# Half 0's strided scores in other banks, constants turned on TensorE, ScalarE's mix ahead of the exponentials, half 7's strided values in two parts

## The chip, the cores and the metric

The kernel runs on one core of a Trainium2 chip. The metric is the device time of one execution in microseconds (us); lower is better. Before and after are each given as the median of three runs on one chip. The engines are named as in the profile: PE is TensorE's matmul, PEld its weight load, DVE is VectorE, ACT is ScalarE, POOL is GpSimd, SP is SyncE, which here only issues transfers. All run their own instruction streams and meet at semaphores.

## What is computed

Sparse attention, then a channel mix, then a gated convolution, all in float32, over 4 batches of 576 tokens, 8 heads of 64:

```python
rel = pos[:, None] - pos[None, :]
mask_local = (rel >= 0) & (rel < 32)                                # heads 0-3
mask_strided = (rel >= 0) & (pos[None, :] % 32 == pos[:, None] % 32)  # heads 4-7
attn = softmax(where(mask, q @ k.T / 8, -1e9)); x = attn @ v        # (4, 576, 512)

x_prev = x shifted by one token
xk = mu_k * x + (1 - mu_k) * x_prev
xr = mu_r * x + (1 - mu_r) * x_prev
k = relu(xk @ w_k); r = sigmoid(xr @ w_r)
x = r * (k * k @ w_v)

h = relu(x @ w_in)                                                  # (4, 576, 1024)
out = (h * sigmoid(conv3(h, conv_w))) @ w_out
```

## The kernel before

A batch is worked in two halves of 288 tokens, so there are eight halves, h = 0 to 7 (NH = 8). Attention and mix of the halves are interleaved by a plan written out by hand: while PE does the mix of half h, it does the attention of half h + 1 in between. The mix of a half has 20 slots. Slots 0 to 7 are the tiles of x_k w_k, slots 8 to 11 those of x_r w_r, slots 12 to 19 the product with w_v, two slots for each of its four tiles. Half 0 multiplies plain float32; the later ones split each operand in a high and a low part and use three products for each (L663 to L665, and L714 to L716), so a tile is 12 matmuls of 288 columns. PLAN and SECOND (L67, L68) say in which slot of the mix PE does scores, ACT exponentials, DVE the normalization and PE the values: for the local block of the next half slots 1, 2, 4, 8, for the strided block 4, 5, 9, 12 (half 1: 2, 3, 5, 7 and 5, 6, 9, 11).

Each engine's program is one loop over halves and slots. In a slot PE first does the attention steps that stand there and then the mix (L746 to L751). Values and scores are very small matmuls: a strided block of an odd half is 88 matmuls in program order, each of which the chip runs as two, with a weight load each. The banks of tiles are a ring of four: tile t waits until ACT has done the ReLU of tile t - 4, that is `relu_done` at FT * h + t - 3 (L675). ACT does for each of the first eight tiles a ReLU, a square and the cast to the high part (L828, L832, L836), for the next four the sigmoid (L842). It also casts the mixed inputs (high_xk L848, high_xr L854) and does the exponentials (L817), one for each score tile, 9 in a local block, 11 in a strided one. ACT's functions lie in tables; where exponentials follow the sigmoids of the half before, a table is loaded (ACT_TABLE_LOAD). In ACT's loop (L897 to L916) the order in slot s is: exponentials, high_xr in slots 1 and 3, then the mix of tile s - 1.

The start stands outside the loops. PE warms up with matmuls of zeros (keep_warm, L720), turns q and k of half 0 (turn_rows), does the three score blocks (L730, L731, L734), the values (L736, L737, L741), and between the last of them the first products of the mix (plain_w_k, L649). DVE masks the scores and takes their maxima (mask_and_max, L1004), lays k out (lay_k, L1150), and turns the constants mu_k, mu_r and conv_w (rows_c to cols_c, L1163). ACT lays q out, and copies the strided values of half 0 (L894). The strided scores of half 0 are in banks 4 and 5 as the local ones are, so PE waits for the maxima of these (L533).

Transfers: SP issues, in this order, rows of q for half 0, V for the local heads, four loads of w_k of 512 KB each, rows of half 1, w_v and w_r, then the V rows of half 1 (L365 to L379). POOL issues the constants and 18 of the 24 loads of the strided V rows of half 0 (L461), ACT the other six (L884). At the end of the attention of half 7 POOL loads the next weights (L503) and SP x2 (L397); the gated convolution follows as a loop.

Of the kernel before, what the change touches and what calls it, by code (L numbers as in the profile page):

```python
# [10 lines left out]
P = 128  # L11
# [5 lines left out]
def attention_channel_mix_gated_conv(  # L17
# [17 lines left out]
    HG = H // 2  # L35
# [41 lines left out]
    WARM_START, WARM_COLS, WARM_SLOT = 23, 224, 4  # L77
# [14 lines left out]
    with ExitStack() as ctx:  # L92
# [32 lines left out]
        BW = 3  # L125
# [58 lines left out]
        const_loaded, const_turned = sem("const_loaded"), sem("const_turned")  # L184
# [16 lines left out]
        o_done, o_copied, first_copied = sem("o_done"), sem("o_copied"), sem("first_copied")  # L201

# [157 lines left out]
        def _(sp):  # L360
# [67 lines left out]
        def _(pool):  # L428
# [32 lines left out]
            load_v_strided(pool, 0, 0, range(1, HG))  # L461
# [60 lines left out]
        def _(pe):  # L522
            def scores(h, i):
# [9 lines left out]
                wait(pe, maxed, tiles_at(h, i) if h or kind == STR else 0)  # L533
# [20 lines left out]
            def values(h, i):  # L554
# [8 lines left out]
                if kind == STR and first == 0:  # L563
                    if h > 1:
                        wait(pe, vs_loaded[c], 16 * VS_DMAS * (h // 2))
                    else:
                        wait(pe, vs_first[c], 16 * (VS_DMAS if c else VS_DMAS - VS_DMAS // HG))
                        if not c:
                            wait(pe, vs_head, 16 * VS_DMAS // HG)
# [25 lines left out]
                else:  # L595
                    order = side_by_side(kind, first, tiles)
                    for two in (order[n:n + 2] for n in range(0, tiles, 2)):
# [13 lines left out]
                mm.then_inc(o_done, 1)  # L611

            def attention(h, slot):
                for i in of_slot(h, 3, slot):
                    values(h, i)
# [118 lines left out]
            scores(0, 2)  # L734
            keep_warm(2 * WARM_SLOT)
# [74 lines left out]
        def _(act):  # L810
# [76 lines left out]
            exps(0, 1)  # L887
            exps(0, 2)

            act.wait_ge(o_done, block_at(1))  # L890
            for pair in range(PAIRS):
                for which in range(2):
                    src, dst = strided_out(0, (pair,), which)
                    copied = nc.scalar.copy(dst, src)  # L894
                copied.then_inc(first_copied, 1)

            for h in range(NH):  # L897
                for slot in range(SLOTS):
# [7 lines left out]
                    if slot >= 1:  # L906
                        mlp(h, slot - 1)
# [65 lines left out]
        def _(dve):  # L973
# [74 lines left out]
            def attention(h, slot):  # L1048
                for i in of_slot(h, 3, slot):
                    copy_out(h, i)  # L1050
# [251 lines left out]
```

## Time and profile before

| | us |
|---|---|
| median of three runs | 531.36 |
| lowest, highest | 530.97, 531.49 |
| the profiled execution | 531.16 |
| its span, first to last instruction | 529.3 |
| PE busy | 517.5 |
| mean granted TensorE clock | 0.997 of full speed |

A profiled execution gives, for each instruction, when it started and how long it took, and what ended the idle time of its engine before it ("issue" where the engine waited for nothing that the profile shows). Lines L... are lines of the kernel before. Matmul durations overlap, since matmuls are pipelined.

### The profile page before, as it was taken

What the parts mean: (1) busy time and instruction counts of PE and PEld (TensorE: products, weight loads), DVE (VectorE), ACT (ScalarE), POOL (GpSimd) and SP (SyncE); (2) the same over time, 40 slices, a digit from 0 to 9 for tenths busy, and PEclk for the clock granted to TensorE, in tenths of its full rate; (3) what the DMA queues carried; (4) which work ended last, traced back from release to release, by engine and by line L of the source; (5) the groups of instructions that cost most, each with busy time, mean ns of one, the idle gap of its engine ahead of it and who ended that gap; (6) DMA issues with size and microseconds to landing.
All of it is one profiled execution on the core that took longest, in us unless ns stands there. A gap on an engine that the chain in (4) does not pass through costs nothing.

```text
span 529.3 us, 15349 instructions
## 1 busy us (share of the span) xinstructions
PE 517.5 (98%) x6200; PEld 480.2 (91%) x6203; DVE 325.3 (61%) x815; ACT 287.8 (54%) x783; POOL 119.3 (23%) x145
## 2 busy tenths in 40 slices
PE   7799999999999999999989999999999999999997
PEld 6477999999999999999989999988998899889985
DVE  5769985658658566657644745883397039807910
ACT  4389288296394592690970724761474048416720
POOL 9229972022031040140221682000000000000000
PEclk9999999999999999999998999999999999999999
DMA  9983423343243341332106126001300130010011
GB/s 203 191 276 56 72 76 63 65 94 65 62 90 65 94 70 41 82 63 45 48 2 249 46 80 213 4 0 61 109 1 12 68 109 0 19 61 0 0 40 59
DMA packets 98622, 39.07 MB, mean 74 GB/s; under 512 B 90952, under 2 KB 91134, under 8 KB 98558
## 3 DMA queue, kind: packets, MB, share of 16 engines
q1 hardware_dynamic: 93992, 33.09, 25.3%
q0 software_dynamic: 1824, 4.44, 2.6%
q10 hardware_dynamic: 2742, 0.66, 0.8%
q8 instruction: 44, 0.72, 0.6%
q14 instruction: 20, 0.16, 0.1%
HBM read 28.72 MB, written 9.44 MB: 72 GB/s over the span
## 4 chain that ended last, share of the span: by engine, by line
PE 85%; DVE 5%; ACT 3%; POOL 3%; issue 2%; DMA 1%; POOLq 0%; DVEq 0%; ACTq 0%
PE ps L769 19%; PE ps L779 19%; PE ps L663 8%; PE ps L664 8%; PE ps L665 8%; PE ps L714 6%; PE ps L715 6%; PE ps L716 6%; PE ps L608 2%; PE ps L550 2%; POOL vs L356 2%; ACT sm L817 2%; DMA vs<-in_v_dram 1%; PE ps L592 1%; DVE diff L1065 1%
## 5 line engine op out<-in xcount | busy, mean ns | idle before, releaser
L486 POOL TENSOR_TENSOR k_lo<-k,k_hi 128x288 fp32r<-128x288 f32 x64 | 60.9, 956 | 192.2 <-ACT k_hi L836 192.2
L1243 DVE SCALAR_TENSOR_TENSOR cbuf<-hbuf,cols_c,cbuf 128x576 f32<-128x576 f32 x64 | 52.4, 819 | 63.5 <-ACT cbuf L939 62.4
L714 PE MATMUL ps<-k_hi,wb_hi 128*128 128x288 f32 x256 | 76.8, 300 | 0.0
L715 PE MATMUL ps<-k_lo,wb_hi 128*128 128x288 f32 x256 | 76.2, 298 | 0.0
L716 PE MATMUL ps<-k_hi,wb_lo 128*128 128x288 f32 x256 | 76.1, 297 | 0.0
L663 PE MATMUL ps<-xk_hi,wa_hi 128*128 128x288 f32 x224 | 67.0, 299 | 0.0
L664 PE MATMUL ps<-xk_lo,wa_hi 128*128 128x288 f32 x224 | 66.1, 295 | 0.0
L665 PE MATMUL ps<-xk_hi,wa_lo 128*128 128x288 f32 x224 | 66.1, 295 | 0.0
L779 PE MATMUL ps<-wb_hi,g_hi 128*128 128x512 f32 x144 | 57.5, 399 | 0.0
L779 PE MATMUL ps<-wb_hi,g_lo 128*128 128x512 f32 x144 | 56.8, 394 | 0.0
L779 PE MATMUL ps<-wb_lo,g_hi 128*128 128x512 f32 x144 | 56.5, 392 | 0.0
L769 PE MATMUL ps<-x_hi,wa_lo 128*128 128x288 f32 x256 | 55.0, 296 | 0.0
L769 PE MATMUL ps<-x_hi,wa_hi 128*128 128x288 f32 x256 | 54.9, 296 | 0.0
L769 PE MATMUL ps<-x_lo,wa_hi 128*128 128x288 f32 x256 | 54.3, 293 | 0.0
L817 ACT ACTIVATE sm<-sm,nb 128x64 f32<-128x64 f32 (+1 forms) x160 | 52.1, 327 | 1.0 <-DVE nb L1009 0.9
L714 PEld LDWEIGHTS ps<-k_hi,wb_hi 128*128 128x128 f32 x256 | 48.9, 191 | 0.3
L715 PEld LDWEIGHTS ps<-k_lo,wb_hi 128*128 128x128 f32 x256 | 48.9, 191 | 0.1
L716 PEld LDWEIGHTS ps<-k_hi,wb_lo 128*128 128x128 f32 x256 | 48.7, 190 | 0.0
L854 ACT CAST xr_hi<-mixed 128x288 fp32r<-128x288 f32 x28 | 11.4, 431 | 62.9 <-DVE mixed L1086 62.9
L966 ACT COPY ob<-ps 128x512 f32<-128x512 f32 x18 | 10.6, 587 | 63.0 <-PE ps L779 62.9
L663 PEld LDWEIGHTS ps<-xk_hi,wa_hi 128*128 128x128 f32 x224 | 42.2, 188 | 0.9
L664 PEld LDWEIGHTS ps<-xk_lo,wa_hi 128*128 128x128 f32 x224 | 42.2, 188 | 0.0
(107 smaller groups left out, 1166.5 us busy)
## 6 DMA issues: line engine op xcount, KB each, us to landing
x2d<-x2s SPq DMA_DIRECT2D x8, 576.0 KB, 3.1
x2raw<-x2d SPq DMA_DIRECT2D x4, 1152.0 KB, 5.5
out_dram<-ob SPq DMA_DIRECT2D x16, 256.0 KB, 2.0
raw<-in_q_dram SPq DMA_DIRECT2D x96, 36.0 KB, 2.0
raw<-in_k_dram SPq DMA_DIRECT2D x96, 36.0 KB, 1.9
wk_raw<-in_moe_w_k_dram SPq DMA_DIRECT2D x4, 512.0 KB, 9.2
wv_raw<-in_moe_w_v_dram SPq DMA_DIRECT2D x4, 512.0 KB, 5.1
ws<-in_moe_w_in_dram POOLq DMA_DIRECT2D x4, 512.0 KB, 7.3
```

The lines of the kernel that those rows point to most:

```text
L486: nc.gpsimd.tensor_tensor(k2_lo[:, m], k2[:, m % K2RING], k2_hi[:, m].bitcast(F32), ALU.subtract).then_inc(k2_done, 1)
L663: nc.tensor.matmul(dst, w_hi(t), x_hi(t), start=(t == 0), stop=False)
L664: nc.tensor.matmul(dst, w_hi(t), x_lo(t), start=False, stop=False)
L665: mm = nc.tensor.matmul(dst, w_lo(t), x_hi(t), start=False, stop=(t == KT - 1))
L714: nc.tensor.matmul(dst, wb_hi[:, f, cols], k2_hi[:, f, :], start=(f == 0), stop=False)
L715: nc.tensor.matmul(dst, wb_hi[:, f, cols], k2_lo[:, f, :], start=False, stop=False)
L716: mm = nc.tensor.matmul(dst, wb_lo[:, f, cols], k2_hi[:, f, :], start=False, stop=(f == FT - 1))
L769: mm = nc.tensor.matmul(ps[:, 2 * (m % GRING) + c, 0:HALF], w[:, t, cols], x[:, c, t, :], start=(n == 0), stop=(n == 3 * KT - 1))
L779: mm = nc.tensor.matmul(ps[:, OUT_BANKS[t], :], g[:, f, toks], w[:, f, :], start=(f == 0 and n == 0), stop=(f == FT - 1 and n == 2))
L817: nc.scalar.activation(e, e, ACT.Exp, bias=nb[:, r, a:a + 1], scale=SCALE, accum_out=den[:, r, a:a + 1]).then_inc(exped, 1)
L854: nc.scalar.copy(xr_hi[:, t], mixed[:, t]).then_inc(xr_hi_done, 1)
L1243: nc.vector.scalar_tensor_tensor(out=c, in0=h[:, o:o + S], scalar=conv[:, o, m:m + 1], in1=c, op0=ALU.mult, op1=ALU.add).then_inc(conv_ste ...
```

## The change

There are seven edits.

- The strided scores of half 0 go to banks 1 and 2 (BS_FIRST) instead of 4 and 5, and PE no longer waits for the maxima of the local block ahead of them. DVE lays the strided k out one step earlier, ahead of the mask of the second local block.
- The constants are turned by a matmul against the identity, behind the strided scores, into bank 0, and ACT copies them to cols_c between two blocks of exponentials; the four transposes on DVE go.
- The warm-up is 14 matmuls of 368 columns instead of 23 of 224.
- The last of POOL's three heads of V rows (six loads) is issued by SP, behind the loads of w_k.
- Of the four copies of the strided values of half 0, DVE does the first, ACT three.
- In a slot ACT does the mix of tile s - 1 first, then high_xr, then the exponentials.
- The strided values of half 7 are done in two parts: 48 of the 88 matmuls in slot 12, the other 40 in slot 13, with the first 12 products of w_v between them; DVE copies them out one slot later.

```diff
-    WARM_START, WARM_COLS, WARM_SLOT = 23, 224, 4
+    WARM_START, WARM_COLS, WARM_SLOT = 14, 368, 4
...
+        BS_FIRST, BW, BC = 1, 3, 0
+        CC = HALF
...
-            return ps[:, BS + which, w * at:w * (at + 1)]
+            bank = BS_FIRST if h == 0 and kind == STR else BS
+            return ps[:, bank + which, w * at:w * (at + 1)]
...
+            load_v_strided(sp, 0, 0, range(HG - 1, HG), vs_head)
...
-            load_v_strided(pool, 0, 0, range(1, HG))
+            load_v_strided(pool, 0, 0, range(1, HG - 1))
...
-                wait(pe, maxed, tiles_at(h, i) if h or kind == STR else 0)
+                wait(pe, maxed, tiles_at(h, i) if h else 0)
...
+                    twos = [order[n:n + 2] for n in range(0, tiles, 2)]
+                    if part is not None:
+                        twos = twos[:SET_S // 2] if part == 0 else twos[SET_S // 2:]
...
-                mm.then_inc(o_done, 1)
+                if part != 0:
+                    mm.then_inc(o_done, 1)
...
             scores(0, 2)
+            pe.wait_ge(const_loaded, 16 * 3)
+            nc.tensor.transpose(ps[:, BC, CC:CC + CR], rows_c[:, :], ident[0:CR, 0:CR]).then_inc(const_turned, 1)
...
             exps(0, 1)
+            act.wait_ge(const_turned, 1)
+            nc.scalar.copy(cols_c[:, :], ps[:, BC, CC:CC + CR]).then_inc(const_copied, 1)
             exps(0, 2)
...
-            for pair in range(PAIRS):
-                for which in range(2):
-                    src, dst = strided_out(0, (pair,), which)
-                    copied = nc.scalar.copy(dst, src)
-                copied.then_inc(first_copied, 1)
+            for pair, which in ((0, 1), (1, 0), (1, 1)):
+                src, dst = strided_out(0, (pair,), which)
+                copied = nc.scalar.copy(dst, src)
+                if which:
+                    copied.then_inc(first_copied, 1)
...
-                    if h < NH - 1:
-                        attention(h + 1, slot)
+                    if slot >= 1:
+                        mlp(h, slot - 1)
                     if h and slot in (1, 3):
                         high_xr(h, slot - 1)
                         high_xr(h, slot)
-                    if slot >= 1:
-                        mlp(h, slot - 1)
+                    if h < NH - 1:
+                        attention(h + 1, slot)
...
             mask_and_max(0, 0)
+            lay_k(0, True)
             mask_and_max(0, 1)
-            lay_k(0, True)
-            dve.wait_ge(const_loaded, 16 * 3)
-            for g in range(P // CR):
-                nc.vector.transpose(cols_c[CR * g:CR * g + CR], rows_c[:, CR * g:CR * g + CR]).then_inc(const_turned, 1)
```

ACT's order at the start of a later half (half 1 and on), before. The casts L854 are high_xr of two tiles, L828, L832 and L836 the mix of tile 0 and then of tile 1, L817 table and exponentials of the next half:

```order
L854 CAST xr_hi<-mixed 128x288 [waits tile_done,r_mixed]
L854 CAST xr_hi<-mixed 128x288 [waits r_mixed]
L828 ACTIVATE rt<-ps 128x288 [waits squared,tile_done]
L832 ACTIVATE k<-rt 128x288 [waits k2_done,relu_done]
L836 CAST k_hi<-k 128x288 [waits tile_done,squared]
L817 ACT_TABLE_LOAD
L817 ACTIVATE sm,den<-sm,nb 128x64 [waits negmax]
L817 ACTIVATE sm,den<-sm,nb 128x64 x8
L828 ACTIVATE rt<-ps 128x288 [waits squared,tile_done]
```

The same place after (L847, L851, L855 are the mix, L873 high_xr, L836 the exponentials):

```order
L847 ACTIVATE rt<-ps 128x288 [waits squared,tile_done]
L851 ACTIVATE k<-rt 128x288 [waits k2_done,relu_done]
L855 CAST k_hi<-k 128x288 [waits tile_done,squared]
L873 CAST xr_hi<-mixed 128x288 [waits tile_done,r_mixed]
L873 CAST xr_hi<-mixed 128x288 [waits r_mixed]
L847 ACTIVATE rt<-ps 128x288 [waits squared,tile_done]
L851 ACTIVATE k<-rt 128x288 [waits k2_done,relu_done]
L855 CAST k_hi<-k 128x288 [waits squared]
L836 ACT_TABLE_LOAD
L836 ACTIVATE sm,den<-sm,nb 128x64 [waits negmax]
L836 ACTIVATE sm,den<-sm,nb 128x64 x8
```

The mix of tile 1 has moved from behind the table and the exponentials to a place ahead of them, and so has the mix of tile 4 at the second set; high_xr stands behind the mix of tile 0.

PE's strided values of half 7 (L608), before, with the first product of w_v behind them:

```order
L608 MATMUL ps<-pt,vs 64x27 [waits maxed,o_copied,p_turned,vs_loaded1]
L608 MATMUL ps<-pt,vs 64x27 x67
L608 MATMUL ps<-pt,vs 64x18 x4
L608 MATMUL ps<-pt,vs 64x27 x4
L608 MATMUL ps<-pt,vs 64x18 x4
L608 MATMUL ps<-pt,vs 64x27 x8
L714 MATMUL ps<-k_hi,wb_hi 128x288 [waits k2_done,sig_done]
```

The same place after, up to the second part (L618 the values, L731 to L733 the products of w_v, of which nine more stand between the fifth row and the second part):

```order
L618 MATMUL ps<-pt,vs 64x27 [waits maxed,o_copied,p_turned,vs_loaded1]
L618 MATMUL ps<-pt,vs 64x27 x47
L731 MATMUL ps<-k_hi,wb_hi 128x288 [waits k2_done,sig_done]
L732 MATMUL ps<-k_lo,wb_hi 128x288
L733 MATMUL ps<-k_hi,wb_lo 128x288
```

```order
L618 MATMUL ps<-pt,vs 64x27 [waits maxed,o_copied,p_turned,vs_loaded1]
L618 MATMUL ps<-pt,vs 64x27 x19
L618 MATMUL ps<-pt,vs 64x18 x4
L618 MATMUL ps<-pt,vs 64x27 x4
L618 MATMUL ps<-pt,vs 64x18 x4
L618 MATMUL ps<-pt,vs 64x27 x8
```

Forty of the 88 matmuls have moved behind twelve products of w_v.

SP's loads behind those of w_k, after; before, the rows of q follow w_k directly:

```order
L376 DMA wk_raw<-in_moe_w_k_dram 128x1024 x4
L361 DMA vs<-in_v_dram 9x6x64
L361 DMA vs<-in_v_dram 9x5x64
L361 DMA vs<-in_v_dram 9x6x64
L361 DMA vs<-in_v_dram 9x5x64
L361 DMA vs<-in_v_dram 9x6x64
L361 DMA vs<-in_v_dram 9x4x64
L338 DMA rows<-in_q_dram 96x4x64 [waits rows_turned]
```

All that SP issues afterwards, the V rows of half 1 too, stands six issues later.

## Rows read from the trace of the kernel before

**Rows 1.** Part 1 of the page: busy us, share of the span, instructions, by engine.
```profile
PE 517.5 (98%) x6200; PEld 480.2 (91%) x6203; DVE 325.3 (61%) x815; ACT 287.8 (54%) x783; POOL 119.3 (23%) x145
```

**Rows 2.** Waits of PE: who waited for whom, us in total, times, longest us.
```profile
PE ps L608 <- issue: 2.1, 2, 1.9
...
PE ps L663 <- ACT rt L828: 0.6, 1, 0.6
```

**Rows 3.** Timeline of the start: start us, us, engine, line, operation [idle before <- releaser].
```profile
22.24 0.99 PEld L608 LDWEIGHTS ps<-pt,vs 27*64 27x64 f32 x88 [1.36 <-DMA vs<-in_v_dram]
...
26.14 0.72 PE L649 MATMUL ps<-xk_raw,wk_raw 128*128 128x288 f32 x2 [0.19 <-DVE xk_raw L1070]
```

**Rows 4.** Timeline of the start, transfers as POOL and SP issue them.
```profile
5.78 10.11 POOL L356 DMA_DIRECT2D vs<-in_v_dram x18
...
11.65 8.64 SPq L333 DMA_DIRECT2D rows<-in_k_dram  x3
...
28.07 6.05 SPq L345 DMA_DIRECT2D vl<-in_v_dram  x8
...
34.16 8.79 SPq L356 DMA_DIRECT2D vs<-in_v_dram  x24
```

**Rows 5.** Timeline, scores and values of half 1's local block.
```profile
28.79 0.81 PEld L550 LDWEIGHTS ps<-kT_l,qT 64*32 64x32 f32 x72 [0.39 <-issue]
...
40.00 1.03 PEld L592 LDWEIGHTS ps<-pt,vl 32*64 32x64 f32 x88 [0.39 <-DMA vl<-in_v_dram]
```

**Rows 6.** Timelines of ACT and of PE in half 2's mix.
```profile
104.63 0.41 ACT L828 ACTIVATE rt<-ps 128x288 f32<-128x288 f32 x1
...
105.99 1.28 ACT L817 ACT_TABLE_LOAD   x1
...
119.59 0.40 ACT L828 ACTIVATE rt<-ps 128x288 f32<-128x288 f32 x1
...
105.32 0.40 PE L663 MATMUL ps<-xk_hi,wa_hi 128*128 128x288 f32 x1
...
120.62 0.29 PE L663 MATMUL ps<-xr_hi,wr_hi 128*128 128x288 f32 x1
```

**Rows 7.** Timelines, half 7: a tile's first product, and its ReLU.
```profile
298.25 0.29 PE L663 MATMUL ps<-xk_hi,wa_hi 128*128 128x288 f32 x1
...
300.04 0.41 ACT L828 ACTIVATE rt<-ps 128x288 f32<-128x288 f32 x1 [0.22 <-PE ps L665]
```

**Rows 8.** Timelines, half 1: a ReLU of ACT, and PE's tile 8.
```profile
81.93 0.39 ACT L828 ACTIVATE rt<-ps 128x288 f32<-128x288 f32 x1
...
82.38 0.40 PE L663 MATMUL ps<-xr_hi,wr_hi 128*128 128x288 f32 x1 [0.60 <-ACT rt L828]
```

**Rows 9.** Timelines, bursts of strided values in halves 3, 5 and 7.
```profile
125.48 1.96 PE L608 MATMUL ps<-pt,vs 27*64 27x27 f32 x176
127.37 0.41 PE L714 MATMUL ps<-k_hi,wb_hi 128*128 128x288 f32 x1
...
199.31 1.43 PEld L608 LDWEIGHTS ps<-pt,vs 27*64 27x64 f32 x136 [0.17 <-issue]
201.13 0.54 PEld L608 LDWEIGHTS ps<-pt,vs 18*64 18x64 f32 x40 [0.39 <-issue]
...
273.63 1.72 PEld L608 LDWEIGHTS ps<-pt,vs 27*64 27x64 f32 x167 [0.17 <-issue]
277.31 0.27 PEld L608 LDWEIGHTS ps<-pt,vs 27*64 27x64 f32 x9 [1.96 <-issue]
...
277.64 0.61 PE L714 MATMUL ps<-k_hi,wb_hi 128*128 128x288 f32 x1
```

**Rows 10.** Busy us in a stretch: engines, then PEclk, DMA share, GB/s.
```profile
277.50:280.70 3.20, 3.20 (x22) 3.15 (x19) 2.92 (x7) 0.17 (x1) 1.47 (x3) 0.50 0.22 34
```

**Rows 11.** DMA from 274 to 276, in 40 slices of 0.05 us.
```profile
GB/s 0 0 0 0 0 0 0 0 0 0 0 0 0 328 0 0 0 0 0 0 0 0 0 0 0 0 0 0 0 0 0 0 0 0 0 0 0 0 0 0
```

**Rows 12.** DMA from 198 to 200, in 40 slices of 0.05 us.
```profile
GB/s 10 0 41 420 138 159 184 118 36 0 0 10 36 87 138 184 139 108 41 20 5 26 87 97 108 128 118 92 36 36 36 26 10 10 10 10 5 10 10 10
```

More of the change, by code:

```diff
@@ L124, in attention_channel_mix_gated_conv @@
         BT = ((((0, 1), (2, 6)), ((7, 0), (1, 2))), (((4, 5), (6, 7)), ((6, 7), (4, 5))))
-        BW = 3
+        BS_FIRST, BW, BC = 1, 3, 0
+        CC = HALF
         EARLY_M, EARLY_T = 4, PAIRS
@@ L183, in attention_channel_mix_gated_conv @@
         rows_turned, q_laid, k_laid = sem("rows_turned"), sem("q_laid"), sem("k_laid")
-        const_loaded, const_turned = sem("const_loaded"), sem("const_turned")
+        const_loaded, const_turned, const_copied = sem("const_loaded"), sem("const_turned"), sem("const_copied")
         W1_TILES = KT + KT // 2 + FT // 2
@@ L201, in attention_channel_mix_gated_conv @@
         o_done, o_copied, first_copied = sem("o_done"), sem("o_copied"), sem("first_copied")
+        part_copied = sem("part_copied")
         diffed = sem("diffed")
@@ L552, in scores, with values @@
                 mm.then_inc(s_done, 1)
-            def values(h, i):
+            def values(h, i, part=None):
                 n, c = block_at(h, i), h % 2
@@ L566, in values @@
                     else:
-                        wait(pe, vs_first[c], 16 * (VS_DMAS if c else VS_DMAS - VS_DMAS // HG))
+                        wait(pe, vs_first[c], 16 * (VS_DMAS if c else VS_DMAS - 2 * VS_DMAS // HG))
                         if not c:
-                            wait(pe, vs_head, 16 * VS_DMAS // HG)
+                            wait(pe, vs_head, 16 * 2 * VS_DMAS // HG)
                 wait(pe, p_turned, n + 1)
@@ L596, in values @@
                     order = side_by_side(kind, first, tiles)
-                    for two in (order[n:n + 2] for n in range(0, tiles, 2)):
+                    twos = [order[n:n + 2] for n in range(0, tiles, 2)]
+                    if part is not None:
+                        twos = twos[:SET_S // 2] if part == 0 else twos[SET_S // 2:]
+                    for two in twos:
                         for k in range(1 + c):
@@ L610, in values @@
                                                           start=(k == 0), stop=(k == c))
-                mm.then_inc(o_done, 1)
+                if part != 0:
+                    mm.then_inc(o_done, 1)
             def attention(h, slot):
                 for i in of_slot(h, 3, slot):
-                    values(h, i)
+                    if h == NH - 1 and blocks(h)[i][0] == STR:
+                        values(h, i, 0)
+                    else:
+                        values(h, i)
+                for i in of_slot(h, 3, slot - 1):
+                    if h == NH - 1 and blocks(h)[i][0] == STR:
+                        values(h, i, 1)
                 for i in of_slot(h, 0, slot):
@@ L1049, in attention @@
                 for i in of_slot(h, 3, slot):
-                    copy_out(h, i)
+                    if not (h == NH - 1 and blocks(h)[i][0] == STR):
+                        copy_out(h, i)
+                for i in of_slot(h, 3, slot - 1):
+                    if h == NH - 1 and blocks(h)[i][0] == STR:
+                        copy_out(h, i)
                 for i in of_slot(h, 2, slot):
@@ L1168, in _ @@
             copy_out(0, 1)
-            dve.wait_ge(const_turned, P // CR)
+            dve.wait_ge(const_copied, 1)
             mix_k(0, 0)
@@ L1172, in _ @@
             mix_k(0, 1)
+            dve.wait_ge(o_done, block_at(1))
+            src, dst = strided_out(0, (0,), 0)
+            nc.vector.tensor_copy(dst, src).then_inc(part_copied, 1)
+            dve.wait_ge(part_copied, 1)
             mix_k(0, 2)
```

## The prediction

> **What bounds the kernel now.** I read the page's busy times first: TensorE (PE) is busy 517.5 of 529.3 us [rows 1], so what counts is where PE stands still, runs slowly, or does what need not be done. The list of PE's waits gives the rest [rows 2]: one wait of 1.9 us on "issue" in a burst of strided values (L608), one of 0.6 us on ScalarE (ACT), and a few at the start. The reader should then go to those places in the timelines. The sum is made against the profiled execution, 531.16 us (span 529.3 plus 1.86 around it). It lies 0.20 under the median of 531.36, which I add at the end.
>
> **1. The start (strided scores of half 0 in banks 1 and 2, constants through PE, the copy shared by DVE and ACT, POOL's last head on SP).** In the trace of before, PE reaches the strided values of half 0 at 22.24, after 1.36 us in which its weight loads wait for the V rows [rows 3]. POOL issued 18 of these loads from 5.78 to 15.89 [rows 4], 0.56 each, and 6.3 us after the last one PE went on. With 12 on POOL the last is issued at 12.5 and is there by about 19. The six that move stand on SP behind the four big loads of w_k, and would be there at 21 to 22. The scores start about 0.6 earlier (no wait for the maxima of the local tiles, k copied before the second mask), DVE loses four small transposes, and the copy of pair 0 is shared; together PE could be up to 1.5 us earlier by 26.14 [rows 3], where it waits 0.19 for the mix. Transpose and copy of the constants (one matmul, one small ACT copy) lie under waits of their engines. Fewer but wider warm matmuls have the same 5152 columns, so no time.
>
> That lead meets the next wait. The local values of half 1 start at 40.00, and what came last before them is a DMA, the V rows of half 1; their idle time of 0.39 is the same as that of other bursts, such as the one at 28.79 [rows 5], so PE and data arrive together. These rows are issued by SP at 28.07 and later, in a queue that depends on nothing PE does: SP was held up in it for 8.64 us from 11.65 [rows 4]. So PE arrives 1.1 to 1.5 earlier and waits. The bytes in front are the same, only six more issues are SP's: 24 such took 8.79 [rows 4], 0.37 each, 2.2 for six, but most of it falls where SP is held up anyway. Bounds: from a gain of 1.0 (the V rows come earlier, as POOL's slow loads are fewer) to a loss of 1.7. I take a loss of **0.3**.
>
> **2. ScalarE's mix ahead of the exponentials.** This is the largest term. At half 1 PE waits 0.60 for the fifth ReLU, which stands behind the exponentials: ReLU at 81.93, PE at 82.38, so PE goes on 0.45 after a ReLU starts [rows 8]. Tile 9 of a half needs the sixth ReLU (relu_done at t-3), and that one stays behind both sets of exponentials, before and after.
>
> What changes is when the first set starts. In half 2 of before, ACT does ReLU, square and cast of tile 0 from 104.63, loads its table at once at 105.99, and from there has no idle time up to the sixth ReLU at 119.59 [rows 6]: 2.99 for nine exponentials, four triples of 1.25, 0.67 for two casts, 3.66 for eleven exponentials, the table 1.41. Now tile 1 comes before the table. Its products start at 105.32 [rows 6], and a ReLU starts 1.79 after the first product of its tile (298.25 to 300.04 [rows 7]): 107.11. So ACT stands from 105.88 to 107.11, and as the same work follows, all of it is 1.23 later: sixth ReLU at 120.82, PE at 121.27 where it started tile 9 at 120.62 [rows 6]. That is 0.65 us of PE's time. The two casts of xr fall into ACT's new gap and cost nothing; DVE's part between the two sets moves along with them. Halves 3 to 6 repeat the pattern and I worked each out in this way: 0.50, 0.65, 0.50 and 0.65 (odd halves have narrower exponentials, 3.36 instead of 3.66). In half 1 the 0.60 at tile 8 goes and 0.43 at tile 9 comes, a gain of 0.17. Sum: a loss of 2.95 - 0.17 = **2.8**. The bounds are 0, if ACT's gap were filled by something I don't see, and 3.5. I take the worked-out value, since five rows of five halves fit it.
>
> In half 0 the same reorder delays the exponentials by about 1 us, but PE's tiles there last 1.93 and the sixth ReLU has a us to spare: nothing.
>
> **3. Half 7's strided values in two parts.** The burst starts at 273.63; 167 pairs of weight load and matmul go through in 1.72 us (10 ns a pair), then both wait until 277.31, and the last nine follow [rows 9]. From its start to the first product behind it are 4.01 us; the same burst in half 3 takes 1.89 (125.48 to 127.37) [rows 9]. So 2.1 are lost, and then the granted clock is 0.50 until 280.7 [rows 10], the lower level of 1.2 GHz, after an idle stretch: 3.05 us of products do what 1.5 do at 2.4 GHz. Loss in all 3.6.
>
> What is waited for is the program itself. One packet of 16 KB on the instruction queue starts at 274.65 [rows 11], and the stall ends 2.65 later. In half 5 one starts at 198.15 [rows 12] and a stall of 0.39 ends at 201.13 [rows 9], 2.95 later. Counted through the program (a load and a matmul each, fp32 rows twice, as 44 rows show as 88 matmuls; waits that are instructions of their own too), the two stalls stand before PE's instructions 6850 and 9410: 2560 apart, ten times 256. Blocks of 256 instructions, with one edge at 78 and one at 334 of the 352 in half 7's burst, which runs from the first to the second in 1.3 us, faster than a block comes.
>
> The Trainium skill (Runtime: NRT & Kernel Launch, Instruction fetch mechanics) has blocks of 256 instructions too, but says that crossing one is "mostly hidden" because dispatch is slower than the refill, and gives PE room for 2048 instructions. The trace disagrees: PE stood 1.86 us. By the page the split would gain nothing (rival C).
>
> After the change the program is 16 instructions shorter before this place (nine warm pairs less, one pair more, and waits). The edges stand at 94 and, in the second part, at 131. Time to the second: 96 pairs 1.0, twelve products between 1.7, the switch back 0.3, 65 pairs 0.7, in all 3.7, that is 277.3. The block is there at 277.4 to 277.9: a stall of **0.4** (0 to 0.8). Switching twice costs another **0.5** (0.3 to 0.6: 0.17 idle before the burst [rows 9], the first product 0.40 long instead of 0.29 [rows 6], and the array emptied). An idle time of 0.4 has lowered no clock here. Gain 3.6 - 0.9 = **2.7** (1.2 if the clock still falls, 3.3 at best). The copy out is not earlier than before, but its readers have over 10 us.
>
> **4. Half 5 pays for the shift.** Its edges move from 16 and 272 to 32 and 288 of the burst. The first one is crossed later by 16 instructions, and if PE's queue is then still among products at 0.13 a pair, that is 1.06 us, against 0.08 if it is in the burst. The second is reached 0.08 later. So the stall grows by 0 to 1.0; I take **0.6**.
>
> Sum: 0.3 + 2.8 + 0.6 - 2.7 = +1.0; 531.16 + 1.0 = 532.2, and 0.2 for the median: about **532.3**.
>
> **Rivals.**
> A, as above: 532.3, own range 531.2 to 533.5.
> B, ACT's new order costs nothing: tile 9 doesn't wait, because ReLU 1 starts sooner or the exponentials wait for something else that also moves. Then 532.3 - 2.8 = 529.5, faster. For it speaks that 0.58 us of slack were there at tile 9; against it, that ACT had no gap in which the delay could vanish.
> C, the stall of half 7 is not one of program blocks and stays: the split costs its 0.5, half 5 doesn't change. 532.3 + 2.7 + 0.5 - 0.6 = 534.9. Against it: the two stalls are a whole number of blocks apart.
> D, V rows of half 1 land earlier, and 1.0 to 1.3 of the lead stay: about 531.0.
> E, slower by another 1.5: the clock falls to 1.2 GHz behind a longer idle time. Half 5's stall decides: at 1.9 us of idle it fell, at 0.39 it didn't [rows 9, 10], and I expect 0.9 to 1.4. The wait at 40.0 is of that size too. 533.8.
>
> **How the numbers follow.** A 0.55, B 0.16, C 0.07, D 0.11, E 0.11. The forecast is A's 532.3. Leaving out a tenth at either end, mostly part of B below and C above, the range is 529.6 to 534.2. A difference of 0.2% (1.06 us) is about what a measurement of this kernel can tell from no change, so faster ends at 530.3 and slower begins at 532.4. Faster: most of B and a little of D, 0.17. Slower: C, E and half of A, 0.43. Within: the rest, 0.40.
>
> **What would show it.** In the profile of after: a wait of PE on ACT's ReLU of about 0.6 at tile 9 of halves 1 to 6 and none at tile 8 of half 1 (step 2); ACT idle about 1.2 ahead of the second ReLU of a half; no wait over 0.8 in half 7's values and a granted clock of 1.00 behind them (step 3); a longer "issue" wait in half 5's (step 4); a wait of PE for the V rows at about 40 (step 1). If there is no wait at tile 9, I am wrong by nearly three us; if the start of half 1's local values is at 38.7, by one.

## The result, and the profile of the changed kernel

The changed kernel took 533.39 us (median; the single times go from 531.67 to 534.62), the kernel before 531.36. The ratio is 1.0034, with an interval of 1.0023 to 1.0046: slower by 0.34%, 1.8 us (the medians as they stand differ by 2.0). The profiled execution is one of 533.80 (span 532.0); against the 531.16 of the one before, 2.64 us are to be explained.

PE's waits, as before in [rows 2] (engine, tile and line <- what it waited for: us in total, times, longest):

```profile
PE ps L680 <- ACT rt L847: 3.2, 6, 0.6
PE ps L599 <- issue: 1.6, 2, 1.0
PE ps L739 <- POOL warm L435: 1.3, 1, 1.3
PE ps L618 <- issue: 1.2, 3, 0.6
PE ps L599 <- DVE mx L1025: 0.4, 1, 0.4
```

Read it against the old list. One wait for a ReLU has become six (L680 is the first line of a product, L847 the ReLU). The 1.9 us on "issue" in the strided values (now L618) are gone, a few smaller ones are there. A wait for DVE's maxima (L1025) is new. It stands before the local values of half 1, which [rows 5] has at 40.00:

```profile
40.79 1.13 PE L599 MATMUL ps<-pt,vl 32*64 32x32 f32 x88 [0.42 <-DVE mx L1025]
```

ACT in half 2 (start, us, engine, line, operation [idle before <- releaser]), where [rows 6] has the same stretch of before:

```profile
105.45 0.41 ACT L847 ACTIVATE rt<-ps 128x288 f32<-128x288 f32 x1 [9.63 <-PE ps L682]
...
108.14 0.41 ACT L847 ACTIVATE rt<-ps 128x288 f32<-128x288 f32 x1 [0.67 <-PE ps L682]
...
109.51 1.28 ACT L836 ACT_TABLE_LOAD   x1
...
121.88 0.39 ACT L847 ACTIVATE rt<-ps 128x288 f32<-128x288 f32 x1
```

The idle time of 0.67 before the second ReLU and the two casts of xr, 0.67 as well, are the gap of ACT that was foretold. The sixth ReLU starts 16.43 after the first; before it was 14.96 (104.63 to 119.59). And PE, at the ninth tile counted from 0, goes on 0.44 after it:

```profile
122.32 0.40 PE L680 MATMUL ps<-xr_hi,wr_hi 128*128 128x288 f32 x1 [0.62 <-ACT rt L847]
```

Its first product is 0.40 long, like the one behind each wait for a ReLU at a clock of 1.00; those behind it take 0.29.

The long bursts of strided values, PE's weight loads. First half 5, then half 7 in its two parts; [rows 9] has them before:

```profile
202.72 1.54 PEld L618 LDWEIGHTS ps<-pt,vs 27*64 27x64 f32 x144 [0.17 <-issue]
204.98 0.44 PEld L618 LDWEIGHTS ps<-pt,vs 27*64 27x64 f32 x32 [0.72 <-issue]
```
```profile
279.00 1.05 PEld L618 LDWEIGHTS ps<-pt,vs 27*64 27x64 f32 x96 [0.17 <-issue]
281.89 0.76 PEld L618 LDWEIGHTS ps<-pt,vs 27*64 27x64 f32 x66 [0.16 <-issue]
282.95 0.32 PEld L618 LDWEIGHTS ps<-pt,vs 27*64 27x64 f32 x14 [0.31 <-issue]
```

Half 5 stands before pair 144, where the count had put an edge (instruction 288), for 0.72 instead of 0.39. Half 7 stands before pair 66 of its second part (the count said 131 instructions, 65.5 pairs) for 0.31 instead of 1.96. Behind it the clock is full, where [rows 10] had 0.50 (stretch, busy us of PE, PEld, DVE, ACT, POOL, then PEclk, DMA share, GB/s):

```profile
283.40:286.60 3.20, 3.20 (x25) 3.20 (x26) 3.06 (x7) 0.43 (x1) 1.64 (x3) 1.00 0.29 44
```

Where the 2.64 went, from the start of the first product of a tile in both traces: up to half 1's first tile 0.85 later (0.3 there before 40 us, 0.4 in the wait for the maxima, the rest behind it); tiles 8 to 11 of halves 1 to 6 together 4.14 (0.88, 0.72, 0.89, 0.71 and 0.88 in halves 2 to 6, 0.06 in half 1); half 5's stall 0.33; half 7 -2.76. That is 2.56; the last 0.1 is rounding and the end of the kernel.

One thing more is different in this execution: the granted clock is 0.50 from 16.9 to 20.3, where it was 1.00 before. Three of the twelve executions of the changed kernel have a mean clock as low as this one's, 0.997; the other nine have 0.999 or 1.000.

### The profile page after: what moved, and what is told of

It is laid out like the page before. It is cut to its first block, busy times and chain, and to the rows that moved or that the text cites. A ratio compares the mean times of both kernels' runs of the same rounds, so it can differ in the third digit from the quotient of the medians.

```text
span 532.0 us, 15336 instructions
## 1 busy us (share of the span) xinstructions
PE 520.8 (98%) x6195; PEld 479.8 (90%) x6195; DVE 325.8 (61%) x812; ACT 287.6 (54%) x783; POOL 114.3 (21%) x139
## 4 chain that ended last, share of the span: by engine, by line
PE 81%; ACT 15%; issue 2%; DVE 1%; POOL 0%; ACTq 0%; POOLq 0%
PE ps L788 19%; PE ps L798 19%; ACT sm L836 7%; PE ps L731 7%; PE ps L732 6%; PE ps L733 6%; PE ps L680 5%; PE ps L681 4%; PE ps L682 4%; PE ps L666 3%; PE ps L618 2%; ACT k L851 2%; ACT rt L847 2%; PE ps L739 2%; PE ps L556 2%
## 5 line engine op out<-in xcount | busy, mean ns | idle before, releaser
L492 POOL TENSOR_TENSOR k_lo<-k,k_hi 128x288 fp32r<-128x288 f32 x64 | 59.8, 937 | 199.8 <-ACT k_hi L855 199.5
L731 PE MATMUL ps<-k_hi,wb_hi 128*128 128x288 f32 x256 | 76.1, 297 | 0.0
L733 PE MATMUL ps<-k_hi,wb_lo 128*128 128x288 f32 x256 | 75.5, 295 | 0.0
L680 PE MATMUL ps<-xk_hi,wa_hi 128*128 128x288 f32 x224 | 67.0, 299 | 0.0
L847 ACT ACTIVATE rt<-ps 128x288 f32<-128x288 f32 x64 | 25.8, 404 | 67.5 <-PE ps L682 67.5
L798 PE MATMUL ps<-wb_hi,g_hi 128*128 128x512 f32 x144 | 57.5, 399 | 0.0
L836 ACT ACTIVATE sm<-sm,nb 128x64 f32<-128x64 f32 (+1 forms) x160 | 52.1, 327 | 0.3 <-DVE nb L1030 0.3
L731 PEld LDWEIGHTS ps<-k_hi,wb_hi 128*128 128x128 f32 x256 | 48.1, 188 | 0.3
L733 PEld LDWEIGHTS ps<-k_hi,wb_lo 128*128 128x128 f32 x256 | 48.1, 188 | 0.0
L680 PEld LDWEIGHTS ps<-xk_hi,wa_hi 128*128 128x128 f32 x224 | 42.1, 188 | 0.9
```

Source lines behind the costliest of these rows:

```text
L492: nc.gpsimd.tensor_tensor(k2_lo[:, m], k2[:, m % K2RING], k2_hi[:, m].bitcast(F32), ALU.subtract).then_inc(k2_done, 1)
L680: nc.tensor.matmul(dst, w_hi(t), x_hi(t), start=(t == 0), stop=False)
L731: nc.tensor.matmul(dst, wb_hi[:, f, cols], k2_hi[:, f, :], start=(f == 0), stop=False)
L733: mm = nc.tensor.matmul(dst, wb_lo[:, f, cols], k2_hi[:, f, :], start=False, stop=(f == FT - 1))
L798: mm = nc.tensor.matmul(ps[:, OUT_BANKS[t], :], g[:, f, toks], w[:, f, :], start=(f == 0 and n == 0), stop=(f == FT - 1 and n == 2))
L836: nc.scalar.activation(e, e, ACT.Exp, bias=nb[:, r, a:a + 1], scale=SCALE, accum_out=den[:, r, a:a + 1]).then_inc(exped, 1)
```

## Experiments

Theory 1 was, after this reading: the new order of ACT costs 4.5 us in all, the split of half 7 wins 2.6, because a block of the program then has time to arrive, and the start wins nothing. The rival was in most runs that one of these prices belongs to something else. Each part was first taken out or done alone. The medians of before lay between 530.9 and 531.9 in these comparisons, so each is told by its ratio to the kernel before that ran beside it.

**ACT's order taken out of the changed kernel.**

```diff
-                    if slot >= 1:
-                        mlp(h, slot - 1)
+                    if h < NH - 1:
+                        attention(h + 1, slot)
...
-                    if h < NH - 1:
-                        attention(h + 1, slot)
+                    if slot >= 1:
+                        mlp(h, slot - 1)
```

> The changed kernel with ScalarE's order of before put back (exponentials ahead of the mix), all else as changed. Theory 1: the order costs all of what the traces show at tiles 8 to 10 of halves 1 to 6 (0.73 to 0.89 each, less the 0.67 won at tile 8 of half 1: 4.1) and the 0.4 of wait at 40.8 in the start. Time 533.39 - 4.5 = 528.9, no wait of PE on the ReLU but half 1's 0.6. Theory 2: it costs the 2.8 that the prediction worked out, the rest of the waits are there for another reason (the shifted program, the start): 530.6.

528.32, ratio 0.9933 (0.9915 to 0.9952). The prediction's 2.8 for the order would have left 530.6, above the slowest time here (529.28), and the nearest ends of this interval and the changed kernel's are 3.8 us apart. PE's waits have one ReLU again, and none for the maxima:

```profile
PE ps L599 <- issue: 1.6, 2, 1.0
...
PE ps L618 <- issue: 0.9, 2, 0.7
PE ps L680 <- ACT rt L847: 0.6, 1, 0.6
```

**The kernel before with the new order alone** (the same edit the other way).

> The kernel before with the new order of ScalarE alone. Theory 1: slower by the same 4.1 at tiles 8 to 10, and by 0 to 0.4 at the start, since the wait for the maxima may lie beside the one for the V rows there: 531.36 + 4.1 to 4.5 = 535.5 to 535.9. Theory 2: 531.36 + 2.8 = 534.2.

535.52, ratio 1.0063 (1.0044 to 1.0082): 3.3 us slower, 2.3 to 4.4 by the interval. The order thus cost 5.4 where it was taken out (1.0034 against 0.9933) and 3.3 where it was put in; the 4.5 of the traces lie between, and the prediction's 2.8 can't be excluded by the second alone. Its trace can: tiles 8 to 11 of halves 1 to 6 cost 4.1 again (0.05 in half 1, then 0.86, 0.72, 0.87, 0.73 and 0.87), in a kernel in which nothing else is changed. Its waits for ReLUs and for the maxima are those of the changed kernel; the other two rows are waits that the kernel before has too:

```profile
PE ps L663 <- ACT rt L828: 3.2, 6, 0.6
PE ps L722 <- issue: 2.8, 3, 2.3
PE ps L608 <- issue: 1.9, 1, 1.9
...
PE ps L592 <- DVE mx L1004: 0.4, 1, 0.4
```

So the wait for the maxima at the start belongs to ACT's order, not to the edits of the start: in the changed kernel half 1's local exponentials end at 36.9 instead of 35.3, DVE normalizes them behind that, and its masks and maxima of the strided tiles, queued behind, end after PE arrives.

**The kernel before with half 7's split alone.**

```diff
-                    for two in (order[n:n + 2] for n in range(0, tiles, 2)):
+                    twos = [order[n:n + 2] for n in range(0, tiles, 2)]
+                    if part is not None:
+                        twos = twos[:SET_S // 2] if part == 0 else twos[SET_S // 2:]
+                    for two in twos:
```

> The kernel before with half 7's strided values in two parts alone (TensorE and VectorE follow). The program ahead of half 7 is unshifted, edges of 256-instruction blocks at 78 of the first part and 115 of the second, half 5's as before (16 and 272). Theory 1 (the stall is the arrival of the program's next block): stall of 0.3 to 0.5, clock 1.00 behind it, gain 2.6: 528.7. Theory 2 (the stall belongs to something else that falls at this time): the stall of about 1.9 stays in the second part or at the products ahead of it, and the extra switching costs 0.3 to 0.5: 531.8.

528.11, ratio 0.9939 (0.9916 to 0.9963), 3.2 us faster, and 3.2 is what half 7 wins in the trace. No stall at all in half 7:

```profile
273.71 1.05 PEld L611 LDWEIGHTS ps<-pt,vs 27*64 27x64 f32 x96 [0.17 <-issue]
276.59 0.97 PEld L611 LDWEIGHTS ps<-pt,vs 27*64 27x64 f32 x80 [0.16 <-issue]
```

That the stall went doesn't yet show that it was one of program blocks. For that, the edges had to be moved with no edit near the bursts.

**78 more instructions of PE, far ahead.**

```diff
+            for _ in range(39):
+                nc.tensor.matmul(ps[0:32, BW, 0:16], warm[:, 0:32], warm[:, 0:16], start=True, stop=True)
             for m in range(EARLY_M):
                 plain_w_k(m, (0,))
```

> The kernel before with 39 tiny matmuls (32 x 16, into the warm bank, 78 instructions) ahead of the first plain product, where TensorE waits 0.79 and then 0.91 anyway. Nothing else is changed. By the count the edges of the long bursts move to 96 and 352 in half 1, 132 in half 3, 194 in half 5, 0 and 256 in half 7. Theory 1 (blocks of 256 instructions, a second edge too soon behind a first): half 5's stall of 0.39 goes, half 7's of 1.96 is at 256 and under 0.5, its clock stays 1.00; 531.36 - 0.4 - 3.3 = 527.7. Theory 2 (a burst of 352 is too long in itself, or the stall belongs to its time): both stay, 531.4 to 531.8.

534.69, ratio 1.0051 (1.0030 to 1.0073): slower, and yet the strongest sign for the blocks. Half 7 runs through (first row), though its burst is as long as ever, and half 5 too. In half 1, where the count had an edge at 352, right behind the last of the 352 instructions, the first product behind the burst waits 1.96 (rows 2 and 3), where before there was none:

```profile
281.11 1.86 PEld L608 LDWEIGHTS ps<-pt,vs 27*64 27x64 f32 x176 [0.17 <-issue]
```
```profile
53.60 1.86 PEld L608 LDWEIGHTS ps<-pt,vs 27*64 27x64 f32 x176 [0.39 <-issue]
57.42 2.90 PEld L649 LDWEIGHTS ps<-xr_raw,wr_raw 128*128 128x128 f32 x7 [1.96 <-issue]
```

The clock is 0.51 from 57.5 to 60.5. And the padding itself paid at its place in the start, where transfers are dense; the clock is 0.50 behind this wait too, from 22.9 to 26.3:

```profile
22.86 0.32 PE L740 MATMUL ps<-warm 128*32 128x16 bf16 x6 [3.35 <-issue]
```

By half 1's first tile 8.0 us are lost; behind it the trace wins 4.1 (0.5 in half 5, 3.6 in half 7), as theory 1 had it. The theory that a long burst is the cause falls here; what I had missed is that the other bursts and the start have edges too.

The traces show the edges directly. Number TensorE's records from 0 in program order (weight loads, matmuls, and the waits and register instructions of its sequencer). Leaving aside the 0.2 to 0.4 ahead of each change from one kind of work to another, the waits that no semaphore explains stand before records 449, 6849 and 9409 in the kernel before, 450, 706, 6849 and 9410 in the changed one, and 449, 705 and 1985 here: each a multiple of 256 plus 193 or 194. The traces of the two kernels and of the twelve runs have 37 waits of over 0.2 at such places, and each ends 2.3 to 3.0 us after a packet of 16 KB on the instruction queue starts: in the kernel before 198.18 to 201.13 and 274.67 to 277.31, here 20.09 to 22.86 and 55.15 to 57.42.

**The edits of the start alone** (the changed kernel without the other two parts).

> The edits of the start alone: the changed kernel with ScalarE's order of before and half 7's strided values in one piece. Edges of the long bursts at 32 and 288 in half 5, at 94 and 350 in half 7. Theory 1 (blocks): half 5's stall grows from 0.4 to 0.8, half 7's stall stays near 1.9 and stands before the last pair of the burst, the clock falls behind it; the start itself is 0 to 0.3 slower. Time: before + 0.4 to 0.8. Theory 2 (the start's edits are worth a us, and e1 was fast for that): before - 0.8.

532.50, ratio 1.0021 (0.9999 to 1.0044), which by itself can't be told from no change. In the trace the first tile of half 1 stands where it stood before (-0.02), half 5 loses 0.37 and half 7 another 0.21, as theory 1 has it. Half 7's stall has moved with the program, by 16 instructions: in [rows 9] it stood behind 167 pairs, here behind 175, before the last one:

```profile
273.88 1.84 PEld L618 LDWEIGHTS ps<-pt,vs 27*64 27x64 f32 x175 [0.17 <-issue]
277.88 0.15 PEld L618 LDWEIGHTS ps<-pt,vs 27*64 27x64 f32 x1 [2.17 <-issue]
```

In the start, the strided values of half 0 stood until 22.24 for the V rows [rows 3]. Here PE is earlier at that place and stands longer, to 22.29:

```profile
18.65 1.75 PEld L666 LDWEIGHTS ps<-xk_raw,wk_raw 128*128 128x128 f32 x8 [1.25 <-issue]
22.29 1.00 PEld L618 LDWEIGHTS ps<-pt,vs 27*64 27x64 f32 x88 [1.88 <-issue]
...
39.99 1.03 PEld L599 LDWEIGHTS ps<-pt,vl 32*64 32x64 f32 x88 [0.51 <-DMA vl<-in_v_dram]
```

The row names no releaser, but the trace has one: the last of the semaphore updates of the six V loads that now stand on SP is at 22.23, 0.06 earlier. POOL's twelve were there by about 19.4 (that is their last update in the changed kernel), SP's six were issued by 11.9 and took until then behind the four loads of w_k. In before the last of all was at 22.20. So the loads moved away from POOL arrive as late as they did from POOL.

**96 more instructions by waits among products.** Waits that are already satisfied lengthen the program with little work.

```diff
                     mm = nc.tensor.matmul(dst, w_lo(t), x_hi(t), start=False, stop=(t == KT - 1))
+                    if pads:
+                        for _ in range(8):
+                            pe.wait_ge(warm_set, 1)
```

(pads is true in tiles 1 to 6 of half 1.)

> The kernel before with waits that are already satisfied, eight behind each group of products in tiles 1 to 6 of half 1, which the program has as 96 more instructions of TensorE (edges: 174 in half 1's long burst as before, 114 in half 3's, 176 in half 5's, 238 in half 7's: no burst holds two). The padding of the first try cost 3.4 by its own place in the start; here it lies among products, of which each takes 0.13 us. Theory 1 (blocks): both stalls gone as there, none new, clock 1.00 in half 7: before - 3.9, plus 0 to 0.6 for the waits. Theory 2 (what the first padding won in halves 5 and 7 came from its delays in the start and not from the edges): before + 0 to 0.6.

529.29, ratio 0.9964 (0.9951 to 0.9978): faster, but by 1.9 instead of 3.3 or more. (The trace is of the slowest of its ten executions, 531.49, with a start 2.6 slower.) Halves 5 and 7 have no stall; half 3 has a new one, in the products behind its burst, where the count has an edge 18 instructions past the end. Behind the start the trace has +0.4 in half 1 (1.0 for the waits, less the 0.6 of PE's wait for the ReLU), +1.4 in half 3, -0.5 in half 5 and -3.6 in half 7:

```profile
132.88 0.29 PE L720 MATMUL ps<-k_hi,wb_lo 128*128 128x288 f32 x1 [1.22 <-issue]
```

**ACT's new order at the strided block alone (slot 5).**

```diff
+                    early = h and slot == 5
+                    if early:
+                        mlp(h, slot - 1)
                     if h < NH - 1:
                         attention(h + 1, slot)
...
-                    if slot >= 1:
+                    if slot >= 1 and not early:
                         mlp(h, slot - 1)
```

> The kernel before, with ScalarE's mix ahead of the exponentials in slot 5 of halves 1 to 6 alone (the strided block): the first block stands where it stood, behind tile 0. Theory 1 (the loss of the new order is the gap before the second ReLU, which moves everything behind it by the length of a tile): the fifth ReLU comes ahead of the exponentials at 114.7 in half 2, the sixth stays at 119.6, so no wait at tile 9 and the 0.6 at tile 8 of half 1 is gone: before - 0.65. Theory 2 (any delay of the strided exponentials delays tile 9, or the strided values behind them): slower by 1 or more.

531.32, ratio 1.0006 (0.9989 to 1.0024). Neither theory is quite right. Halves 2 to 6 lose nothing, as theory 1 has it. In half 1 the gain failed: the wait at tile 8 is gone (3.42 us from tile 7 to tile 8 became 2.75), and stands at tile 9 instead:

```profile
84.44 0.40 PE L663 MATMUL ps<-xr_hi,wr_hi 128*128 128x288 f32 x1 [0.47 <-ACT rt L828]
```

In half 1 ACT's first ReLU starts 3.25 behind PE's first tile (2.83 in the kernel before), in half 2 1.89; ACT is simply late, and the order only chooses which tile pays.

**The last two together.**

> The two together, the padding by waits and the mix ahead of the strided exponentials alone. If both theories hold, before - 4.5 or so (less 0 to 0.6 for the waits), 527.2, faster than the kernel before and the changed one. If the padding doesn't act, before - 0.6.

528.86, ratio 0.9961 (0.9946 to 0.9976), 2.1 us faster where 4.5 had been expected, and the same as the padding by itself within the intervals. Half 3's stall is there again, 0.65 long.

**77 more instructions instead of 96** (seven waits in place of eight).

> The kernel before with seven instead of eight satisfied waits behind each group of products in tiles 1 to 6 of half 1: 77 more instructions. Edges: 174 in half 1's long burst, 133 and 389 in half 3's (389 is 37 past its end), 195 in half 5's, 1 and 257 in half 7's. With 96 more, half 3 had 114 and 370, and 0.8 to 1.2 were lost in the products behind that burst. Theory 1 (two edges have to be some 3.7 us apart as TensorE's queue takes them; 370 came 2.7 after 114, 389 comes 3.7 after 133): no stall over 0.2 behind the start; the waits cost 0.8, of which 0.6 lie in the wait for the fifth ReLU of half 1. Before - 3.6. Theory 2 (the stall in half 3 came from something else that the waits do): it stays at about 1, before - 2.8.

527.81, ratio 0.9927 (0.9907 to 0.9948): the fastest of all here, and faster than both kernels of this case. Halves 3, 5 and 7, each in its turn:

```profile
125.73 1.86 PEld L608 LDWEIGHTS ps<-pt,vs 27*64 27x64 f32 x176 [0.17 <-issue]
```
```profile
199.78 1.86 PEld L608 LDWEIGHTS ps<-pt,vs 27*64 27x64 f32 x176 [0.17 <-issue]
```
```profile
273.60 1.36 PEld L608 LDWEIGHTS ps<-pt,vs 27*64 27x64 f32 x129 [0.17 <-issue]
275.18 0.65 PEld L608 LDWEIGHTS ps<-pt,vs 27*64 27x64 f32 x47 [0.22 <-issue]
```

Nineteen instructions fewer took most of half 3's stall away: at the edge, 37 instructions behind the burst, 0.2 are lost instead of 1.4 and 0.8. The 0.22 in half 7 stands behind pair 129; the edge at 257 is there. The expected price of the waits themselves didn't come: no tile of half 1 is later by them, and PE's wait of 0.6 for the fifth ReLU is still there.

**ACT's new order at the local block alone (slot 2).**

> The kernel before with ScalarE's mix ahead of the exponentials in slot 2 of halves 1 to 6 alone (the local block), the counterpart of the run that did it in slot 5 alone. Theory 1 (the loss is ScalarE's gap ahead of the second ReLU, which delays all behind it by 1.2 to 1.3): tile 8 of halves 2 to 6 waits 1.1 for the fifth ReLU, tile 9 nothing or 0.1 more, half 1 about 1.2 more than its 0.6: slower by 1.1 x 6 = 6.6, at least 5. Theory 2 (it takes both moves to lose): within 1 of before.

550.57, ratio 1.0364 (1.0333 to 1.0396): 19 us slower, three times the forecast. Two things came on top of the delay that I had counted. The strided exponentials wait for DVE (first row), whose maxima stand behind the local block's normalizing; in the complete new order the fifth ReLU fills that time. And the waits at tile 8, of 2.03 to 2.18 us, are so long that the clock falls behind them in halves 3 to 6 (from tile 8 to tile 9 are 2.20 to 3.04 us there, 1.70 in half 2). The rows behind the first are half 2's and half 3's wait and the stretches behind them:

```profile
119.82 0.35 ACT L817 ACTIVATE sm<-sm,nb 128x64 f32<-128x64 f32 x1 [0.95 <-DVE nb L1012]
```
```profile
123.92 0.40 PE L663 MATMUL ps<-xr_hi,wr_hi 128*128 128x288 f32 x1 [2.18 <-ACT rt L828]
```
```profile
163.30 0.61 PE L663 MATMUL ps<-xr_hi,wr_hi 128*128 128x288 f32 x1 [2.03 <-ACT rt L828]
```
```profile
124.00:126.00 2.00, 2.00 (x15) 2.00 (x16) 1.93 (x4) 1.91 (x6) 0.81 (x1) 1.00 0.45 73
163.40:165.40 2.00, 2.00 (x9) 2.00 (x10) 1.91 (x4) 1.91 (x6) 0.80 (x1) 0.50 0.33 52
```

**The split, and 18 more instructions.** (The split as above, four waits behind the groups of tiles 1 and 2 of half 1.)

> The kernel before with half 7's strided values in two parts and 18 more instructions in tiles 1 and 2 of half 1 (satisfied waits). Edges: 174 in half 1's long burst, 194 in half 3's, 0 and 256 in half 5's, 62 of the first part and 99 of the second in half 7. Theory 1: half 5's stall of 0.4 is gone as well as half 7's of 3.6, the switching costs 0.4, the waits lie in half 1's wait: before - 3.6, no issue wait over 0.3 behind the start. Theory 2 (0 and 256 only went well together with the other padding): half 5's stall stays or grows, before - 2.6 to - 3.0.

(Sixteen of the 18 instructions are waits in half 1, two come with the split.) 528.42, ratio 0.9944 (0.9926 to 0.9963), 3.0 us faster. Half 7 has 0.31 before its second edge. Half 5's stall is gone (its next tile 0 stands 37.65 behind half 4's, 37.92 before), but this is not to be told from the split alone (0.9939).

**The start's edits without any stall behind them.** (The run with the start alone, and the 96 instructions.)

> The changed kernel without two of its parts (ScalarE's order is that of before, half 7's strided values are in one piece) and with 96 more instructions in tiles 1 to 6 of half 1 (satisfied waits), so that the long bursts have their edges at 190, at 130 and 386, at 192, and at -2 and 254: what is left is the start, without any stall of the program behind it. Theory 1 (the edits of the start win nothing, since the program's blocks come at 15 to 16 and at 22.3 whatever TensorE has ready): the same as the kernel before with 77 more instructions, that is before - 3.5 to - 3.9, values of half 1 at 40.0 to 40.3, with issue waits of 1.0 to 1.6 at the local or strided values of half 0. Theory 2 (the start's edits are worth up to 1 us): before - 4.5 to - 4.9, local values of half 1 at 39.0. Theory 3 (the start's edits lose 0.8 to 1.2, as the median of the run with them alone could mean): before - 2.5 to - 3.

527.90, ratio 0.9937 (0.9915 to 0.9959). Within its interval it equals the 77 instructions on the kernel before (0.9927). The interval alone, -2.2 to -4.5, leaves theory 3 its -2.5 to -3 and touches theory 2's; against both speaks the trace, with half 1's local values at 40.18 and its first tile 0.17 later than before. But theory 1 gave the wrong reason for a right time. The strided values of half 0 wait 2.38, and not for a block of the program, whose edge lies 63 instructions into this burst. The last update of SP's V loads is at 22.47:

```profile
22.53 1.01 PEld L618 LDWEIGHTS ps<-pt,vs 27*64 27x64 f32 x88 [2.38 <-issue]
```

## Why the prediction was right, and where it was not

The forecast was 532.3 in a range of 529.6 to 534.2, with slower the likeliest of three chances; 533.39 came. The miss is nearly all in one term, ACT's order. Point by point:

**ACT's order (2.8 forecast).** The mechanism was the one described, tile 9 and the sixth ReLU, and tile 8 of half 1 freed. It cost 4.14 at the tiles and 0.42 at the start. Two terms of the sum were too small. The second ReLU starts 1.90 after its tile's first product (106.24 to 108.14), where I had taken 1.79 from half 7, whose tiles follow on each other without scores between; so the sixth is 1.36 later in the half, not 1.23. And a tile behind a wait takes longer by 0.1 (tile 9 to 10 1.68, before 1.59), its first product being 0.40. That is 0.2 a half in halves 2 to 6, 1.1 together, and with half 1, which lost 0.06 instead of winning 0.17, 1.4 in all. The third was a step that failed: "In half 0 the same reorder delays the exponentials ... nothing". I had followed the delay to ACT's ReLU only. It goes on through DVE, from the exponentials to the normalizing and to the maxima queued behind it, and stops PE at 40.8 for 0.42.

**The split (2.7 forecast).** 2.76 in the traces of the two kernels, 3.2 by the run with it alone (2.0 to 4.5 by the interval) and in its trace. The stall was 0.31, within the 0 to 0.8 given. Rival C, that it isn't one of program blocks, is out: the stall moved by eight pairs when the program became 16 instructions shorter, went from half 7 to half 1 with 78 more, and stood in each trace where the count had an edge. The page's rule that such crossings are mostly hidden (the Trainium skill, Runtime: NRT & Kernel Launch, Instruction fetch mechanics) holds for the bulk of the edges here: of some 49 in the program before, three have a wait over 0.3. It fails where tiny matmuls take PE from one edge to the next in 1.3 us, 1.96 lost in half 7, and in the start, 3.35 lost with the first padding.

**Half 5 (0.6 forecast).** 0.33. It stalled at the place that was named, for 0.72. Rival E had expected 0.9 to 1.4 there; the clock stayed at 1.00.

**The start (0.3 forecast).** 0.3 came, but by another way, and that the number fits is luck: in the three traces that have these edits without ACT's order, half 1's first tile is 0.11, -0.02 and 0.17 later than before. I had said that PE would have a lead of 1.1 to 1.5 at 26.14 and lose it at 40.00 to the V rows of half 1. The lead was lost at 22 already, to those of half 0: I had them on SP "at 21 to 22", and they came at 21.4 to 22.5. Where they came early, as in the changed kernel's own trace (21.45), PE was late for another reason: 0.56 at 16.33, inside the local values and behind their fifth pair, where the count has an edge 11 instructions in, and then the clock of 0.50 up to 20.3, at which four warm matmuls take 1.89 (1.04 in the last run above):

```profile
16.33 1.87 PE L599 MATMUL ps<-pt,vl 32*64 32x32 f32 x83 [0.56 <-issue]
18.13 1.89 PE L739 MATMUL ps<-warm 128*128 128x512 bf16 x4
```

That PE would be held again at 40 is only half shown: idle there was 0.51 in the run with the start alone, instead of 0.39.

**The sum** would with the measured terms be 0.3 + 4.56 + 0.33 - 2.76 = 2.4 for the profiled executions, and 0.1 more of the start's that I can't place; the medians differ by 2.0, since the profiled one of after lies 0.4 above its median and that of before 0.2 below.

What stays open is how much of the spread between executions of one kernel (529.2 to 534.6 for the start alone) comes from the first 25 us. The traces name two causes, but no run fixed either. One is when the block that begins before record 449 comes: its packet starts at 12.5 in the kernel before and PE goes on at 15.0; in the three traces of kernels with the start of before where the packet starts latest, at 13.4 to 14.1, PE goes on at 16.1 to 17.0, the clock then falls, and half 1's first tile is 1.3 to 2.6 later. The other is how often the clock falls. A trace in which it is 0.50 once within the kernel has a mean clock of 0.996 or 0.997, one with two such stretches 0.994; of the 22 executions of before that ran beside the 77 instructions, the ten at 0.997 took 530.5 to 532.3 and the eight below that 532.1 to 534.0.

## What to carry to other kernels

A delay must be followed through every queue that it reaches: one ReLU moved ahead of the exponentials delayed the next ReLUs on ScalarE, but also VectorE's normalizing and the maxima queued behind it, and TensorE paid for both. Before a burst of hundreds of tiny matmuls is taken apart, count where the program's blocks of 256 instructions end in it; padding by 77 instructions of satisfied waits, at a place where the trace shows no cost for them, won 0.7%, as much as the best part of the change. Check the padding against all bursts, since an edge that leaves one may enter another.

## What the runs showed of the hardware

- TensorE's program arrives in blocks of 256 instructions. In a burst of 352, passed at 10 ns a pair, the second of two edges lies 1.3 us behind the first, and the wait there grows with how deep in the burst they lie: edges at 0 and 256 none to 0.06, 1 and 257 0.22, 16 and 272 0.01 to 0.39, 32 and 288 0.72 to 0.82, 78 and 334 1.65 to 1.99, 94 and 350 2.17 us. With edges at 114 and 370, behind the burst's end (by the rows some 2.7 us apart), it was 0.65 and 1.22, with 133 and 389 (some 3.7) 0.1.
- A block's packet is 16 KB, and where TensorE stood for one, it went on 2.3 to 3.0 us after the packet's start.
- In the start, where transfers are dense (mean DMA share 0.75 from 18.5 to 22.9), a block was waited for 3.35 us.
- Loads issued by SP behind 2 MB of weights landed some 10 us after their issue (issued by 11.9, there at 21.4 to 22.5). PE's wait for them is shown as "issue" in two traces: the word covers waits for several semaphores too.
- Satisfied waits that lengthen the program by 96 instructions cost some 1.0 us among products, of which 0.6 lay in another wait; those that lengthen it by 77, one fewer behind each group, delayed nothing. Why the step is so sharp, no run here shows.
- The granted clock fell to 0.50 (1.2 of 2.4 GHz) behind idle times of PE of 1.54, 1.86, 2.03, 2.06 and 2.17 us and more, in the changed kernel's start behind 1.04 and 0.56 close together, and stayed at 1.00 behind others of 1.66, 1.96, 2.03 and 2.18. One length doesn't decide it; what else does, no run here shows.
- Executions of the kernels without a long stall lie closer together (527.3 to 529.6 for the one with 77 more) than those of before (529.1 to 534.0).
